# Experts' blocks: when their rows count as read; a fourth slot in the ring of scores; two weight pieces of the head one beat later

## The reference, cut to what matters

```python
# attention with a window of 128 and a slope by head; (4, 8, 576, 64)
scores = where(mask, q @ k.T / sqrt(D) + bias, -1e9)
x = softmax(scores) @ v                      # then reshaped to (2304, 512)
# a dense MLP, 512 -> 2048 -> 512
r = maximum(x @ w_in, 0);  x = (s * r * r + b) @ w_out
# mixture of 8 experts, 512 -> 1024 -> 512, two experts for each token
noisy = x @ w_gate + log1p(exp(x @ w_noise)) * noise
top2 = the two largest of noisy; top2_w = softmax over the two
for e in range(8):
    for k in range(2):
        mask = top2[:, k] == e
        out[mask] += top2_w[mask, k] * (maximum(x[mask] @ w1[e], 0) @ w2[e])
```

## Time and profile before

| | us |
|---|---|
| median of 3 runs | 1229.83 (1229.63 to 1230.3) |
| the profiled execution | 1228.59 |
| its span, first to last instruction | 1226.8 |
| TensorE busy | 1088.4 (89%) |
| VectorE busy | 661.0 (54%) |
| ScalarE busy | 480.1 (39%) |
| GpSimd busy | 126.5 (10%) |

### The profile page before, as it was taken

How to read it: one execution, slowest core, us unless ns; L and a number is a source line. 1 busy time by engine, 2 the same in 40 slices (tenths; PEclk the granted TensorE clock), 3 DMA queues, 4 the chain that set the end, 5 groups by cost and what they waited for, 6 DMA issues and landing times.

```text
span 1226.8 us, 18393 instructions
## 1 busy us (share of the span) xinstructions
PE 1088.4 (89%) x5845; PEld 948.0 (77%) x5846; DVE 661.0 (54%) x1967; ACT 480.1 (39%) x988; POOL 126.5 (10%) x130
## 2 busy tenths in 40 slices
PE   5699899999999999999478898889789789789795
PEld 4588789889899888898377787778578578578594
DVE  6777567767676766547654354435235235235222
ACT  7666455555464565354232232223123123123110
POOL 0000000200200200102211012100100101101111
PEclk9799899999999999999789998989889889889898
DMA  6479933432522421325343143415215224223212
GB/s 194 130 237 338 307 98 96 155 91 83 164 78 78 147 87 50 106 87 171 134 127 111 58 153 95 147 33 171 72 45 169 80 66 168 77 80 111 71 43 86
DMA packets 80146, 146.96 MB, mean 120 GB/s; under 512 B 12748, under 2 KB 13388, under 8 KB 80080
## 3 DMA queue, kind: packets, MB, share of 16 engines
q1 hardware_dynamic: 70640, 125.91, 32.4%
q0 software_dynamic: 9440, 20.22, 4.7%
HBM read 109.31 MB, written 47.57 MB: 128 GB/s over the span
## 4 chain that ended last, share of the span: by engine, by line
PE 76%; issue 6%; DMA 5%; DVE 5%; ACT 5%; SPq 1%; POOL 0%; ACTq 0%; DVEq 0%; POOLq 0%
PE bank L1208 22%; PE bank L1209 21%; PE bank L1210 21%; DMA rows<-rows_scratch 4%; PE bank L1189 3%; PE bank L1176 2%; PE bank L1327 1%; PE bank L1234 1%; PE bank L1155 1%; ACT x_sc L583 1%; PE bank L1362 1%; PE bank L1320 1%; PE bank L1156 1%; DMA stage_a<-in_w_second 1%; ACT g_hi L751 1%
## 5 line engine op out<-in xcount | busy, mean ns | idle before, releaser
L1208 PE MATMUL bank<-w_hi,g_hi 128*128 128x512 f32 x312 | 134.4, 431 | 1.0
L1209 PE MATMUL bank<-w_lo,g_hi 128*128 128x512 f32 x312 | 128.1, 411 | 0.0
L1210 PE MATMUL bank<-w_hi,g_lo 128*128 128x512 f32 x312 | 127.3, 408 | 0.0
L643 ACT ACTIVATE relu<-bank 128x384 f32<-128x384 f32 x96 | 47.1, 490 | 164.4 <-PE bank L1210 157.1
L739 ACT ACTIVATE g_hi<-bank 128x384 fp32r<-128x384 f32 x64 | 31.5, 492 | 170.9 <-PE bank L1210 168.1
L843 DVE SCALAR_TENSOR_TENSOR relu<-relu,sb_scale 128x384 f32<-128x384 f32 x96 | 59.3, 618 | 69.0 <-ACT relu L643 68.0
L506 POOL DMA_INDIRECT rows_scratch<-x,slot x36 | 38.6, 1071 | 531.7 <-DVE x L924 522.5
L1076 DVE SCALAR_TENSOR_TENSOR g_lo<-bank,g_hi 128x384 fp32r<-128x384 f32 x64 | 35.6, 556 | 82.9 <-ACT g_hi L739 76.0
L583 ACT ACTIVATE x_sc<-x_sc,least 128x256 f32<-128x256 f32 (+1 forms) x144 | 69.9, 488 | 20.0 <-DVE least L788 19.8
L837 DVE TENSOR_TENSOR w_now_lo<-stage_a,w_now_hi 128x1024 fp32r<-128x1024 f32 x48 | 58.7, 1223 | 30.7 <-ACT w_now_hi L637 28.1
L1327 PE MATMUL bank<-ident,rows 128*128 128x128 f32 x72 | 19.1, 418 | 62.9 <-DMA rows<-rows_scratch 62.9
(11 more groups left out here) (202 smaller groups left out, 2889.3 us busy)
## 6 DMA issues: line engine op xcount, KB each, us to landing
stage_a<-in_w_first SPq DMA_DIRECT2D x92, 256.0 KB
stage_a<-in_w_second SPq DMA_DIRECT2D x92, 256.0 KB
qk_raw<-in_qk SPq DMA_DIRECT2D x144, 128.0 KB, 2.7
y_scratch<-x SPq DMA_DIRECT2D x21, 768.0 KB, 9.1
stage_b<-in_w_first SPq DMA_DIRECT2D x28, 256.0 KB
stage_b<-in_w_second SPq DMA_DIRECT2D x28, 256.0 KB
rows_scratch<-x SPq DMA_DIRECT2D x24, 258.0 KB, 8.0
rows<-rows_scratch SPq DMA_DIRECT2D x8, 774.0 KB, 6.7
```

The lines of the kernel that those rows point to most:

```text
L643: act.activation(relu[:, (t * C1 + c) % GR, :], h_bank[c % 2][:, 0:TOK1], ACT.Relu).then_inc(relu_ready, 1)
L1208: pe.matmul(psum, lh, rh, start=(first and n == 0), stop=False)
L1209: pe.matmul(psum, lh, rl, start=False, stop=False)
L1210: done = pe.matmul(psum, ll, rh, start=False, stop=(last and n == len(pairs) - 1))
```

## The change

Four edits. `XS`, the number of slots of `x_sc`, goes from 3 to 4. In the head, VectorE's two `rest_of_weights` come one beat later, behind beats 13 and 14; ScalarE's rounding of the same weights and SyncE's loads keep their places. In a tile, `meta_used` is incremented by an instruction behind the eight index steps at c == 2, and no longer by the write of `out_to` at c == 4. In a block, `b_meta_used` is incremented behind the eight index steps, and no longer by the write of `out_to_1`. The writes of `out_to` and `out_to_1` stay where they are.

```diff
--- before.py
+++ after.py
@@ -46,7 +46,7 @@
 WEIGH = 6
 LEAD = 4 * (BLK1 - 1) + WEIGH + 1
 FREE = 12
-XS = 3
+XS = 4
 VS = 3
 SROUNDS = C1 + (T1 - 1) * (C1 // 2) + C2
 NOWHERE = float(1 << 20)
@@ -940,8 +940,8 @@
                 rest_of_qk(0, 1)
                 for i in range(LEAD):
                     head_beat(i)
-                    if LEAD - 3 <= i < LEAD - 1:
-                        rest_of_weights(i - (LEAD - 3), i - (LEAD - 3))
+                    if LEAD - 2 <= i < LEAD:
+                        rest_of_weights(i - (LEAD - 2), i - (LEAD - 2))
                 dve.wait_ge(const_in, CONSTS * 16)
                 dve.wait_ge(const_done, 4)
                 for t in range(T1):
@@ -1080,10 +1080,10 @@
                             dve.wait_ge(rows_in, e * 16 + 16)
                             indices(meta, e, rows[:, :, DM:RW], BLK2, region[:, 0, bass.ds(e, 1)], y_from[:])
                             dve.sem_inc(meta_ready, 1)
+                            dve.sem_inc(meta_used, 1)
                         if c == 4:
                             dve.wait_ge(out_done, e * (BLK2 * 16))
-                            dve.tensor_scalar(out_to[:], sought[:, 1, :], NOWHERE, None, ALU.add
-                                              ).then_inc(meta_used, 1)
+                            dve.tensor_scalar(out_to[:], sought[:, 1, :], NOWHERE, None, ALU.add)
                         if more:
                             rest_of_later(e * C2, c, other + c)
                     if later:
@@ -1102,13 +1102,14 @@
                     dve.wait_ge(b_rows_in, i * 16 + 16)
                     indices(b_meta, i, rows_1[:, :, DM:RW], 1, start_f[:, bass.ds(i, 1)], y_from_1[:])
                     dve.sem_inc(b_meta_ready, 1)
+                    dve.sem_inc(b_meta_used, 1)
                     for half in range(2):
                         cols = slice(half * DM, (half + 1) * DM)
                         dve.wait_ge(b_gh_ready, i * 2 + half + 1)
                         dve.tensor_tensor(gb_lo[:, cols], b_turned[half][:], gb_hi[:, cols].bitcast(F32), ALU.subtract
                                           ).then_inc(b_gl_ready, 1)
                     dve.wait_ge(b_out_done, i * 16)
-                    dve.tensor_scalar(out_to_1[:], sought[:, 1, 0:1], NOWHERE, None, ALU.add).then_inc(b_meta_used, 1)
+                    dve.tensor_scalar(out_to_1[:], sought[:, 1, 0:1], NOWHERE, None, ALU.add)
                     rest_of_block(i + 1)
                     dve.wait_ge(b_done, i + 1)
                     dve.wait_ge(b_fetched_in, i * 16 + 16)
```

## The result

| | median, us | runs | ratio to before | 95% interval |
|---|---|---|---|---|
| before | 1229.95 | 4 | | |
| changed | 1133.72 (1132.12 to 1136.22) | 4 | 0.9219 | 0.9199 to 0.9239 |

A forecast was written before the change was run, and what follows sets the result against it. It took TensorE's 17 waits for late-requested block rows, and the half clock behind them, as the bound. Profiled 1228.6 - 65.8 - 35.7 - 3.6 + 8.0 = 1131.5, plus 1.2 for the median: 1133 us, range 1121 to 1145.

The forecast's parts named there:

- the stalls, less what stays in first blocks: Experts' stage: TensorE's 17 waits for a block's rows go, 65.8 us, but 8.0 us stay in eight first blocks.
- half clock behind them: Experts' stage: matmuls slowed by the lower clock after each stall return to full speed, 17 x 2.1 = 35.7 us gained.
- head: Head: rest of the weights one beat later lets x_lo and the first MLP product come earlier, 3.6 us gained.
- tile's signal, fourth slot: Tile's row load and the scores' ring: each worth 0; bounds 0.5 us either way, and 0 to 2 gained.
- The bound and the moved signal: Experts' blocks: late row requests bind; signalling after the eighth index step removes the wait in nine later blocks, slack 1.3 us.
- The rest in first blocks: First block of each expert, eight of 17: a wait of 0.4 to 1.6 us stays, taken as 1.0, 8 us in all.
- rule of ring order: First blocks: the load cannot pass the earlier y write on its queue; residue nearer 1.6 us a block, 13 us.
- Rival A: First blocks: remaining waits of about 1 us still bring the clock down; 17 us more, 1150 us; chance 0.10.
- B: First blocks: loads held by y write and scatters, 3 us of wait plus slow clock, 33 more: 1166 us; chance 0.08.
- C: Blocks: SyncE is held elsewhere, so the change doesn't do what it says; 1226 to 1230 us; chance 0.03.
- D: Blocks: the moved load delays the gather that L1118 needs; slower, 1243 us; chance 0.02.

The follow-up runs named there:

- busy_wait: The kernel before, with 16 extra unread matmuls per block run right ahead of the transposes that wait: 1195.23 us, ratio 0.9731.
- all_but_block: The changed kernel with the block's signal put back; fourth slot, head and tile's signal stay changed: 1223.30 us beside 1227.78, ratio 0.9984.
- xs3_again: The changed kernel with three slots of scores, not four: 1131.05 us beside 1229.93, ratio 0.9195; the changed kernel on that chip 1129.89.
- block_only: The kernel before, with the block's signal alone moved behind the eight index steps: 1138.79 us beside 1228.42, ratio 0.9284.
- stall_1: The changed kernel with the block's signal delayed by an extra VectorE reduction of 936 columns, about 1.0 us: 1149.81 us, ratio 0.9361.
- stall_2: The changed kernel with the block's signal delayed by an extra VectorE reduction of 1872 columns, about 2.0 us: 1188.90 us, ratio 0.9679.
- after_again: The changed kernel once more, unchanged, on another chip: 1129.89 us, ratio 0.9191.

## Why the prediction was right

| term of the sum | forecast, us | measured, us | from |
|---|---|---|---|
| the stalls, less what stays in first blocks | 65.8 - 8.0 = 57.8 | 59.1 | waits 62.9 to 5.3, with 0.17 for each stall that was or is |
| half clock behind them | 35.7 | 33.8 to 35.3 | busy_wait's stage; 94.4 - 59.1 |
| head | 3.6 | 2.1 (2.6 from where the change acts, see below) | first product 57.83 to 55.69 |
| tile's signal, fourth slot | 0 | not told from 0 | all_but_block, xs3_again |
| sum, profiled | 97.1 | 96.5 | 1228.59 to 1132.12 |

**The bound and the moved signal** were right: the gain in the stage is the block's alone (block_only). In later blocks the load left 1.04 us behind the index step (forecast 0.9), and nothing took the wait's place; a later block takes 12.67 us, where the prediction's times for a first one give 12.9 (856.15 to 869.0).

**The rest in first blocks** was forecast as 1.0 us each (0.4 to 1.6) and is 0.66 in the mean, 1.0 at most: inside. The time from y write to load was forecast as 3.7 us; it was 4.45 in the first profile and 3.60 in the second. The Trainium skill's rule of ring order (DMA: Bandwidth & Descriptors, queues, rings and completion order) had pointed to 13 us; 5.3, and 0.8 with a load still nearer to the y write, do not show that price. The rule itself stands untested here: as shown above, the y write had drained 3.2 us behind its issue, ahead of the load's turn. The prediction's 3.7 us between the two were enough for that, and it had not asked how long the write takes.

**The clock** was right in size, and busy_wait shows the cause, which the prediction had only argued. Rival A had the right mechanism at the wrong length: at 1 us the clock stays (stall_1), at 2 us it mostly falls (stall_2). The Trainium skill (TensorE: Matmul & The Clock Gate, section on a second failure mode, the cycling through PSUM queues) tells of a kernel in which frequent short idle times between groups of matmuls made the clock go up and down. This case's traces show the like behind 13 of 17 stalls of about 2 us, and not behind those of up to 1.6 us in stall_1, nor the shorter ones that the change left. Rivals B, C and D are out: no first-block wait over 1.0 us (1.1 in after_again) where B had 3, no other wait of SyncE that holds the load, no wait of L1119 for a gather.

**The head** is the step that came out short, in its size. The prediction let x_lo move "with" the last beat, by 3.6 us. The last beat did: its scores start at 50.28 for 53.67, 3.4 us earlier. But x_lo runs at 54.94 for 57.08, 2.1 us earlier and not at 53.5, and it waits 2.07 us. VectorE, then ScalarE, then TensorE:

```profile
50.28 0.42 DVE L788 CUSTOM_DVE_ANT_0 x_sc<-bank,nbias 128x256 f32<-128x256 f32 x1
...
54.94 0.69 DVE L809 TENSOR_TENSOR x_lo<-bank,x_hi 128x512 fp32r<-128x512 f32 x1 [2.07 <-ACT x_hi L604]
```

```profile
53.31 0.60 ACT L595 ACTIVATE pT<-bank 128x512 f32<-128x512 f32 x1 [1.13 <-PE bank L1190]
...
54.32 0.59 ACT L604 ACTIVATE x_hi<-bank 128x512 fp32r<-128x512 f32 x1
```

```profile
45.88 0.65 PE L1177 MATMUL bank<-ident,x_sc 128*128 128x128 f32 x4 [0.88 <-DVE x_sc L802]
48.39 1.12 PE L1177 MATMUL bank<-ident,x_sc 128*128 128x128 f32 x4 [1.86 <-DVE x_sc L802]
49.53 3.68 PE L1190 MATMUL bank<-pT,v_sb 128*64 128x128 f32 x32
```

x_lo waits for x_hi (L604), that for the copy of L595, and that for TensorE's product of the values (L1190), 3.68 us long at the lower clock, which starts once the transposes at 48.39 are done. TensorE's pause in front of those shrank from 4.0 to 1.86 us, but the clock is at its lower level through the pause and the product in both kernels (granted clock 0.50 from 46.53 to 53.21 now, and from 46.39 to 55.14 before). The chain had moved to TensorE, and the prediction did not ask what was late next there.

Of the missing 1.5 us, 0.5 lies ahead of the edit: the changed kernel's profile comes later to the last transposes in front of it, at 45.88 (above) for 45.40. The ten profiles with the new head come to them at anything from 44.0 to 46.3. These transposes and the MLP's first product, before:

```profile
45.40 0.99 PE L1176 MATMUL bank<-ident,x_sc 128*128 128x128 f32 x4 [0.88 <-DVE x_sc L802]
57.83 0.45 PE L1208 MATMUL bank<-x_hi,w_hi 128*128 128x384 f32 x1 [1.69 <-DVE x_lo L809]
```

The first product after:

```profile
55.69 0.45 PE L1209 MATMUL bank<-x_hi,w_hi 128*128 128x384 f32 x1 [1.76 <-DVE x_lo L809]
```

From those transposes to the first product it is 12.43 us before and 9.81 after, 2.6 less. The same stretch is 12.43 and 12.44 in the two other profiles with the old head (busy_wait, block_only), and 9.6 to 9.8 in all ten with the new one. So the head gives 2.6 to 2.9 us and falls 0.7 to 1.0 short of the forecast by the chain on TensorE; a comparison of two single profiles by their first product alone (53.77 to 56.15 in the ten) tells it poorly.

## What to carry to other kernels

Signal that a buffer is free behind the last read of it, not behind the last operation of the step: with one buffer for the next block's rows, each microsecond of delay came straight out of TensorE's time. Price a stall of TensorE with its echo: stalls of 3.7 us cost 2 us more each in slow matmuls, stalls of 1 us nothing more, so a stall need not vanish to give back the second part. When a wait goes, work out the next one on every engine of the chain, TensorE too.

## What the runs showed of the hardware that I had not expected

- Idle stretches of TensorE of 0.95 to 1.6 us left the clock at the upper level 17 times of 17; of 1.9 to 2.7 us brought it to the lower one 13 times of 17, with one of 2.73 us passing and one of 1.92 us not; of 3.5 to 3.9 us always. Near 2 us the length of the stall alone does not settle it.
- 272 matmuls whose result nobody reads made the kernel before 33 us faster.
- The same program's first-block load left SyncE 4.45 us behind the y write in one profiled execution and 3.60 in another, with the DMA instruction itself 0.69 and 0.33 us long. By the packet records the load's first packet came 4.8 to 5.5 us behind the y write's issue in the one and 4.5 to 4.9 in the other, 0.5 us apart in the mean. Which of the transfers under way is behind it was not tried.
- The 768 KB y write, issued as one transfer, had ended 3.2 us behind its issue, ahead of the next load on the same queue each time. Whether a large transfer ahead of a small one is still under way can be read from the queue's packets in the trace.
